# An attention and two expert layers on one core: the attention's loads asked for one kind a step, the output's zeros in four parts in the last batch

## The reference

```python
scores = scale * np.matmul(q, k.transpose(0, 1, 3, 2))     # masked: 64-blocks, block_i >= block_j
attn = softmax(scores); attn_out = np.matmul(attn, v)       # then laid out as x: 2304 x 512
# experts 1: each token goes to its best of 8 experts, up to a capacity of 576 in token order
h = relu(disp[e] @ w1[e]); y = h @ w2[e]; out[i] = gate_w[i] * y[expert_idx[i], pos[i]]
# experts 2: tokens with x @ w_skip > 0 go to their best of 8 other experts, the rest is copied
out[do_compute] = xc + gate_w * (relu(xc @ w1b[e]) @ w2b[e])
```

## Time and profile before

| | us |
|---|---|
| median of 3 runs | 697.74 |
| lowest and highest | 697.29, 698.19 |
| the profiled execution, its own time | 693.78 |
| its span, first to last instruction | 692.2 |
| TensorE busy | 672.9 |
| attention (TensorE's loop over g) | about 5 to 227 |

### The profile page before, as it was taken

The page is one execution under the profiler, slowest core; times in us unless marked ns, Lnnn a source line. Parts: engine busy times, 40 slices in busy tenths (PEclk is TensorE's granted clock), DMA queues, the critical chain, the costliest instruction groups (busy, mean ns, idle before and its releaser), DMA issues.

```text
span 692.2 us, 16809 instructions
## 1 busy us (share of the span) xinstructions
PE 672.9 (97%) x5586; PEld 591.0 (85%) x5587; DVE 362.8 (52%) x1003; ACT 260.2 (38%) x640; POOL 138.8 (20%) x234
## 2 busy tenths in 40 slices
PE   7999999998998989999999999999899999999997
PEld 6888877887886889999899988998799899999996
DVE  3767777876876743357633366434621444411144
ACT  5556556655655112144412234113221343411133
POOL 5100021012003213211122211222222112112112
PEclk9999999999999999999999999999999999999999
DMA  9957558557314248110611149881365688801101
GB/s 181 232 141 198 173 164 236 151 167 240 84 44 161 74 109 313 37 46 25 226 70 47 39 144 332 310 304 46 135 219 189 226 289 314 283 30 46 46 17 33
DMA packets 95614, 105.89 MB, mean 153 GB/s; under 512 B 63757, under 2 KB 63757, under 8 KB 95568
## 3 DMA queue, kind: packets, MB, share of 16 engines
q1 hardware_dynamic: 84608, 81.03, 37.7%
q0 software_dynamic: 8912, 22.36, 10.1%
q10 hardware_dynamic: 2048, 1.87, 1.0%
HBM read 83.44 MB, written 28.63 MB: 162 GB/s over the span
## 4 chain that ended last, share of the span: by engine, by line
PE 90%; issue 2%; DVE 2%; ACT 2%; DMA 1%; ACTq 1%; another core or an unknown queue 1%; DVEq 0%; POOL 0%; SPq 0%; POOLq 0%
PE ps L1437 33%; PE ps L1445 23%; PE ps L1338 7%; PE ps L1289 6%; PE ps L1313 5%; PE ps L1345 4%; PE ps L1269 3%; PE ps L1281 2%; PE ps L1427 2%; PE ps L1415 2%; PE ps L1421 1%; PE ps L1306 1%; ACT probs L1118 1%; ACTq L270 1%
## 5 line engine op out<-in xcount | busy, mean ns | idle before, releaser
L1437 PE MATMUL ps<-xT,w 128*128 128x128 f32 x1344 | 160.3, 279 | 3.1 <-ACT xT L1162 2.5
L1437 PEld LDWEIGHTS ps<-xT,w 128*128 128x128 f32 x1344 | 157.2, 195 | 6.0 <-ACT xT L1162 3.7
L1445 PE MATMUL ps<-w_hi,hT_hi 128*128 128x512 f32 x256 | 104.5, 408 | 0.6 <-DVE hT_lo L980 0.4
L1445 PE MATMUL ps<-w_lo,hT_hi 128*128 128x512 f32 x256 | 100.0, 391 | 0.0
L1445 PE MATMUL ps<-w_hi,hT_lo 128*128 128x512 f32 x256 | 100.0, 390 | 0.0
L980 DVE SCALAR_TENSOR_TENSOR hT_lo<-ps,hT_hi 128x512 fp32r<-128x512 f32 x64 | 44.2, 691 | 104.0 <-ACT hT_hi L1176 101.9
L1176 ACT ACTIVATE hT_hi<-ps 128x512 fp32r<-128x512 f32 x64 | 38.0, 594 | 150.4 <-PE ps L1437 150.4
L1437 PE MATMUL ps<-xT,w_last 128*128 128x128 f32 x704 | 84.1, 276 | 0.2 <-issue 0.2
L1437 PEld LDWEIGHTS ps<-xT,w_last 128*128 128x128 f32 x704 | 81.6, 192 | 1.4 <-issue 0.7
L1118 ACT ACTIVATE probs<-ps,negmax 128x128 f32<-128x128 f32 (+3 forms) x128 | 65.9, 528 | 29.6 <-DVE negmax L741 26.3
L1171 ACT ACTIVATE w_hi<-w2all 128x1024 fp32r (+1 forms) x48 | 47.0, 1046 | 62.6 <-PE ps L1445 57.4
(11 more groups left out here) (173 smaller groups left out, 872.3 us busy)
## 6 DMA issues: line engine op xcount, KB each, us to landing
w2all<-in_moe_w SPq DMA_DIRECT2D x10, 2048.0 KB, 14.6
w<-in_moe_w SPq DMA_DIRECT2D x7, 2048.0 KB, 9.1
rows<-queue POOLq DMA_DIRECT2D x36, 257.0 KB, 3.0
w2all<-in_moe_w SPq DMA_DIRECT2D x16, 512.0 KB, 5.4
w<-in_moe_w SPq DMA_DIRECT2D x12, 512.0 KB, 4.3
w_last<-in_moe_w SPq DMA_DIRECT2D x3, 2048.0 KB
qn<-in_q SPq DMA_DIRECT2D x32, 144.0 KB, 3.6
out<-pad SPq DMA_DIRECT2D x4, 1152.0 KB
```

The lines of the kernel that those rows point to most:

```text
L1437: last = mm(hTp[j // 4][:, j % 4, :], w1s[slot][:, c, j * P:(j + 1) * P], xT[:, c, :], start=(c == 0), stop=(c == DC - 1))
L1445: last = mm(yp, h_[:, j, :].bitcast(f32r), w_[:, j, :].bitcast(f32r), start=(j + n == 0), stop=(j == FC - 1 and n == 2))
```

## The change

SP's loop now runs over the four steps of each pair, and waits in each for the `pv_ready` of that step. It asks for q of pair+2 in n = 0, for k of pair+2 in n = 1, for v of pair+1 in n = 2 and for the quarter of weights in n = 3. The four writes of zeros, one per batch before, are made at steps (12, 3), (13, 3), (14, 0) and (14, 3), given as (pair, n). Nothing else is changed.

```diff
+            CLEARS = [(PAIRS - 4, 3), (PAIRS - 3, 3), (PAIRS - 2, 0), (PAIRS - 2, 3)]
             for pair in range(PAIRS):
                 b, u = pair // NPAIR, pair % NPAIR
-
                 if pair + 2 < PAIRS:
                     sp.wait_ge(qk_transposed, 4 * (pair + 1))
-                    load_qk(pair + 2)
-
-                if pair + 1 < PAIRS:
-                    if pair:
-                        sp.wait_ge(pv_ready, STEPS * pair)
-                    load_v(pair + 1)
-
-                if b < WSLOT - 1:
-                    load_quarter(b, u)
-                if u == NPAIR - 1:
-                    if b == 0:
-                        sp.wait_ge(pad_made, 1)
-                    sp.dma_start(out.rearrange("(o p j) d -> o p j d", o=B, j=XJ)[b, :, :, :],
-                                 pad[0:XP, 0:D].unsqueeze(1).to_broadcast([XP, XJ, D])).then_inc(out_cleared, 16)
+                for n in range(STEPS):
+                    if pair + n:
+                        sp.wait_ge(pv_ready, STEPS * pair + n)
+                    if n == 0 and pair + 2 < PAIRS:
+                        load_qk(pair + 2, ((q, qn, q_loaded),))
+                    if n == 1 and pair + 2 < PAIRS:
+                        load_qk(pair + 2, ((k, kn, k_loaded),))
+                    if n == 2 and pair + 1 < PAIRS:
+                        load_v(pair + 1)
+                    if n == 3 and b < WSLOT - 1:
+                        load_quarter(b, u)
+                    if (pair, n) in CLEARS:
+                        if (pair, n) == CLEARS[0]:
+                            sp.wait_ge(pad_made, 1)
+                        sp.dma_start(out.rearrange("(o p j) d -> o p j d", o=B, j=XJ)[CLEARS.index((pair, n)), :, :, :],
+                                     pad[0:XP, 0:D].unsqueeze(1).to_broadcast([XP, XJ, D])).then_inc(out_cleared, 16)
```

## The result

| | us |
|---|---|
| before, median of 4 runs beside the changed kernel | 697.51 (696.07 to 698.19) |
| changed, median of 4 runs | 704.74 (703.58 to 707.31) |
| ratio, with its 95% interval | 1.0111 (1.0076 to 1.0147) |
| profiled execution: before, changed | 693.78, 705.74 (spans 692.2, 704.1) |

The changed kernel is slower: by 7.2 us in the medians, 7.7 us by the ratio. The forecast was 708.6 us, 11 us slower, so the direction and the range held and the size was too large.

The account below looks back on a forecast made before the run. The prediction took TensorE, busy 97% of the span, to bound the kernel. Terms of 4.4, 2.7 and 3.8 us summed to 10.9, added to the timed median of 697.7 for 708.6 us; range 702.8 to 712.0.

Parts of the forecast that it names:

- Part 1: Attention: q, k and v asked later still arrive before TensorE needs them, hidden by three steps; cost 0.
- Part 2: Expert 0's last quarter, asked after `pv_ready` 15, delays ScalarE's first split and so TensorE; +4.4 us.
- term A: TensorE's stop behind ScalarE's wait for expert 0's last quarter: +4.4 us, bounds 3.8 to 5.7.
- Part 3: End of attention: SP waits until `pv_ready` 63, so the experts' first tiles are asked late; +2.7 us.
- term B: TensorE's wait for the late first tile, less 0.25 us regained: +2.7 us, bounds 2.5 to 3.3.
- Part 4: TensorE's clock falls to half behind each of the two new waits, 1.9 us each.
- term C: Two clock falls behind the new waits: +3.8 us, bounds 0 to 3.8.
- Part 5: Writes of zeros moved to `pv_ready` 51, 55, 56 and 59: cost 0, between -2.0 and +2.0 us.
- R1: Rival: the clock holds after one or both new waits; 705 (none) to 707 us (one fall), chance 0.27.
- R2: Rival: contention grows, the quarter lands slowest and the clear beside the third scatter adds a stop; 711.9 us, chance 0.15.
- R3: Rival: faster, since SP's loads cause the late scores beside the scatters; 694.8 us, chance 0.05.
- R4: Rival: the `pv_ready` wait passes earlier than read, so only term B with its fall stands; 702.3 us, chance 0.05.

Follow-up runs that it names:

- e3: Changed kernel with expert 0's last quarter asked in n = 0 and no `pv_ready` waits in pair 15; 698.00 us against 695.46 before, ratio 1.0022.
- e8: e3 with the zeros asked near their old places (pairs 3, 7, 11 and 14); 687.43 us against 685.85 before, ratio 1.0026.
- e9: The changed kernel run again without edits; 705.95 us against 697.54 before, ratio 1.0102.
- e12: Kernel before with expert 0's last quarter behind `pv_ready` 15 and the first tiles behind `pv_ready` 63; 707.80 us against 697.54, ratio 1.0137.
- e2: Changed kernel without SP's `pv_ready` waits in pair 15, so the first tiles are asked early; 700.81 us against 695.46 before, ratio 1.0069.
- e7: Changed kernel plus 24 unused transpositions in TensorE's wait for the first tile; 704.99 us against 695.46 before, ratio 1.0139.
- e10: e7 repeated beside e9 on one chip; 706.28 us against 697.54 before, ratio 1.0123.
- e1: Changed kernel with expert 0's last quarter (pair 3) asked in n = 0 instead of n = 3; 699.68 us against 695.46 before, ratio 1.0069.
- e4: Kernel before with expert 0's last quarter (pair 3) waiting for `pv_ready` 15; 693.08 us against 685.85 before, ratio 1.0087.
- e5: Kernel before with SP waiting for `pv_ready` 63 ahead of the first tiles' loads; 690.19 us against 685.85 before, ratio 1.0061.
- e11: Kernel before plus unused transpositions, 14 ahead of the first phase's tile 1, 15 behind its last logits; 694.97 us against 697.54, ratio 0.9961.
- e6: Kernel before with the four writes of zeros at the changed kernel's steps; 687.61 us against 685.85 before, ratio 1.0011.

## Why the prediction was right, and where its size was off

**Part 1, q, k and v later, cost 0.** Held in the changed kernel: in its waits q's load holds TensorE only before the first transposition (0.6 us), and neither k's nor v's holds it at all. Whether the spreading costs or wins a microsecond at the scatters stays open (e3, e8, e9 against e12).

**Part 2, term A.** The mechanism was right in each link. Its size was 4.4 us and measured 3.5 us of TensorE's idle time in the profile (3.0 to 3.3 in e2, e7, e9 and e10), since the quarter landed in 4.5 us where I took 4.9, SP sent the second half 0.40 us behind the first where I took 0.62, and ScalarE reached the wait 0.3 us later than before. Undoing it (e1) and doing it alone (e4) show the cause.

**Part 3, term B.** Right: 2.7 forecast, 3.0 us of idle time and 3.1 us of lateness, of which the 0.25 us before `step_pv(63)` comes back. In e7 and e10, where no fall covers it, 0.3 us do. e2 and e5 show the cause.

**Part 4, term C, is the term that was mis-sized.** I charged 1.9 us behind each new stop, 3.8 in all. Behind the first it came, at 1.5 us. Behind the second it came too, at 1.3 us, but the fall that before had at the copy of x, worth 1.6 us, did not: net about +1.2 us in the profiled pair. That a fall has a price was right, though 1.9 us was at the high end: 1.3 to 1.6 us here, and e11 gives 2.7 us for two. That a new one is added to those already there was wrong. The working had looked at the new waits alone and not at what becomes of the old falls behind them.

The profiled pair is kind to the first stop. Its stretch at half clock lasted 3.4 us there and in e10, but twice as long, 6.8 us, in e2, e4, e7, e9 and e12. By lateness against before, the stretch cost 1.4 to 1.6 us in the first two and 2.2 to 2.8 us in the five. Two windows of e9, whose stop ended at 72.47 us:

```profile
72.00:73.00 1.00, 0.53 (x3) 0.53 (x4) 0.47 (x1) 0.42 (x2) 0.00 (x0) 0.50 0.02 5
...
77.00:78.00 1.00, 1.00 (x9) 0.88 (x9) 0.48 (x1) 0.00 (x0) 0.00 (x0) 0.50 0.00 0
```

So 1.9 us for that stop was too little in most traces, and the size of term C came out too large only because of the second stop.

**Part 5, the zeros, cost 0.** Held: e6 gives +0.11% with an interval over 1. The profiled pair seems to say otherwise, with 4.2 us of lateness added over the three scatters. But e9, the same kernel in another execution, has no fall at either place. And the same lateness comes without the change: e11, whose attention is that of the kernel before, is 2.4 us later than before over the first scatter, with a fall of its own at 107 us, and e12, which has before's zeros and loads there, 1.5 us. A pair of traces would have made a cause of this. Executions also differ at the start: e1, e3 and e10 are 1.5 to 1.7 us late by 20 us, e9 3.5 us. The profiled execution of before had neither, which is part of why it was faster than the median of its runs.

**The sum.** With A 3.5, B 3.1 and net C 1.2 it is 7.8 us, against 7.2 in the medians and 7.7 by the ratio. That it meets so closely is in part luck: with the longer stretch of e9 behind the first stop the same sum gives about 9 us, for a kernel that took 7.1 us more by the ratio in that group (5.2 to 9.0).

**The rivals.** R1, falls fewer than charged, at 705 to 707, is where the median (704.7) came nearest, though not for R1's reason: in the profiled execution the clock fell behind both stops. R2 fell (no landing was slow, and the clear stopped nobody in e6). The stretched issues that it names are all of SP's own queue, so they show nothing of the other engines' DMAs. R3 fell: the late scores at the scatters did not go when the loads moved; VectorE's waits for scores that the profile puts down to "remote" are 5.9 us in the changed kernel against 5.2 in the earlier trace rows:

```profile
DVE negmax L745 <- remote: 5.9, 3, 2.2
```

R4 fell, with the split 4 us late. The rule of the Trainium skill cited there ("TensorE: Matmul & The Clock Gate", Why this matters for your kernels) points the way that e11 went, where filling idle gaps won 2.7 us. But it warns of longer gaps than those, 1.85 and 1.78 us, behind which the clock fell in the earlier trace rows; here the measurement decides.

## What to carry to other kernels

When requests are spread out or tied to later events, look for the one consumer that reads early, and for what stands behind the new waits in the issuing queue: a wait in an iteration that asks for nothing still holds back whatever comes next. Sixteen pairs of moved loads cost about 2 us or less here (e3, e8); two single requests cost the rest, or all of it. And a cost that depends on the clock is counted over the whole stretch, old falls included: a new stop can take the place of a later one's fall.

## What was not expected of the hardware

The chips differ: the same kernel before took 685.85 us on one and 695.46 and 697.54 us on two others. The traces from the faster chip (e4, e5, e6, e8) have no row of scores coming late from "remote" at all, where the three scatters stop VectorE for 5 us or more on the others. The stop beside a scatter thus goes with the chip, not with the loads beside it; its cause was not found. In the earlier trace rows VectorE took at 216.61 us the result of a matmul that had ended at 213.17 us:

```profile
212.97 0.20 PE L1294 MATMUL ps<-mask_k,mask_q 64*128 64x64 bf16 x2
```

On that chip TensorE ran into the first tile earlier, and waited 1.0 and 1.4 us for it in e6 and e8.

TensorE's clock fell behind some idle times of 1.8 us and not behind others as long. At the start of the second phase it fell in all 13 traces in which that stop was left unfilled (1.66 to 2.15 us). At the copy of x it fell in four of nine (before, e3, e7, e10), all with stops of 1.77 to 1.98 us; in four of the other five it had fallen behind the first tile, some 17 us earlier. It also fell with hardly any idle time ahead: at 107.2 us in e11, where TensorE had stood for no more than 0.5 us at a time since 95 us.
